# One-core attention and two feed-forward layers: six weight parts loaded and split between the loads of q and k, squares in PSUM, first chunks folded one by one

## What is computed

```python
qn = q / (norm(q, axis=1) + 1e-6); kn = k / (norm(k, axis=1) + 1e-6)   # over the tokens
s = kn.T @ qn / tau                       # 256 x 256
a = exp(s - s.max(-1)); a /= a.sum(-1) + 1e-9
x = v @ a                                 # 6016 x 256
h = x @ w_in
g = (a0 + a1*h + a2*h*h + a3*h**3) / (1 + |b0|*|h| + |b1|*h*h + 1e-6)
x = g @ w_out
h = x @ w2_in
out = (h * clip(h + 3, 0, 6) / 6) @ w2_out
```

## Time and profile before

| | |
|---|---|
| median of 3 runs | 1117.84 us (1117.04 to 1118.7) |
| profiled execution | 1118.82 us |
| its span, first to last instruction | 1117.0 us |
| mean granted TensorE clock | 0.995 |
| TensorE / VectorE / ScalarE / GpSimd busy | 98% / 80% / 78% / 70% |
| loads of q and k end, as TensorE sees it | 48.7 us |
| first `up1` ends, step 0 begins on ScalarE | 55.4 us |
| slot 16 begins on ScalarE | 108.7 us |

### The profile page before, as it was taken

How to read it: one execution, slowest core, us unless ns; L and a number is a source line. 1 busy time by engine, 2 the same in 40 slices (tenths; PEclk the granted TensorE clock), 3 DMA queues, 4 the chain that set the end, 5 groups by cost and what they waited for, 6 DMA issues and landing times.

```text
span 1117.0 us, 16082 instructions
## 1 busy us (share of the span) xinstructions
PE 1098.1 (98%) x5004; PEld 921.7 (83%) x5004; DVE 894.7 (80%) x1286; ACT 868.4 (78%) x1468; POOL 777.9 (70%) x625
## 2 busy tenths in 40 slices
PE   9988799999999999999999999999999999999998
PEld 8887688888888888888888888888888888888887
DVE  6689899987887887888888888888788798787632
ACT  6699888877877887887777877877877787777643
POOL 0279888777776677777777777777677777766643
PEclk9999899999999999999999999999999999999999
DMA  9931010010110010020011011011011010010010
GB/s 346 305 126 20 1 20 1 15 19 1 20 20 1 10 29 1 0 35 3 0 21 17 1 19 19 0 19 19 1 19 20 1 20 1 1 20 1 1 19 20
DMA packets 105465, 33.82 MB, mean 30 GB/s; under 512 B 92982, under 2 KB 98742, under 8 KB 105398
## 3 DMA queue, kind: packets, MB, share of 16 engines
q1 hardware_dynamic: 104832, 32.52, 11.6%
q10 hardware_dynamic: 566, 0.52, 0.1%
HBM read 26.87 MB, written 6.16 MB: 30 GB/s over the span
## 4 chain that ended last, share of the span: by engine, by line
PE 93%; DVE 3%; ACT 2%; POOL 1%; issue 1%; DMA 0%; SPq 0%; DVEq 0%; ACTq 0%
PE H L469 15%; PE H L471 15%; PE H L470 15%; PE YP L470 7%; PE YP L471 7%; PE YP L469 7%; PE OP L471 7%; PE OP L469 7%; PE OP L470 7%; PE OP L502 3%; PE OP L640 1%; PE OP L644 1%; PE OP L642 1%; DVE H L940 0%; ACT SQ L750 0%
## 5 line engine op out<-in xcount | busy, mean ns | idle before, releaser
L416 POOL TENSOR_TENSOR SQ<-SQ,AB 128x512 f32<-128x512 f32 x176 | 231.2, 1314 | 245.3 <-ACT SQ L750 245.0
L430 POOL TENSOR_TENSOR g_lo<-R,g_hi 128x512 fp32r<-128x512 f32 (+1 forms) x191 | 243.1, 1273 | 28.8 <-ACT g_hi L782 28.8
L422 POOL TENSOR_TENSOR g_lo<-SQ,Y 128x512 fp32r<-128x512 f32 (+1 forms) x192 | 244.9, 1276 | 6.1 <-DVE SQ L970 6.0
L748 ACT ACTIVATE AB<-H,absb 128x512 f32<-128x512 f32 x176 | 121.4, 690 | 142.7 <-PE H L471 142.7
L933 DVE TENSOR_TENSOR T<-T,H 128x512 f32<-128x512 f32 (+1 forms) x192 | 129.1, 672 | 79.2 <-ACT T L756 78.5
L948 DVE SCALAR_TENSOR_TENSOR g_hi<-H,coef,Y 128x512 fp32r<-128x512 f32 (+1 forms) x192 | 141.5, 737 | 58.1 <-ACT Y L769 57.3
L469 PE MATMUL H<-vT_hi,wf_hi 128*128 128x512 f32 (+1 forms) x384 | 149.9, 390 | 8.8 <-DVE SQ L970 4.7
L976 DVE SCALAR_TENSOR_TENSOR R<-R,H 128x512 f32<-128x512 f32 (+1 forms) x192 | 128.1, 667 | 35.3 <-ACT R L775 35.2
L775 ACT ACTIVATE R<-H 128x512 f32<-128x512 f32 (+1 forms) x192 | 113.4, 591 | 51.9 <-PE H L471 51.0
L469 PE MATMUL YP<-g_hi,wd_hi 128*128 128x512 f32 (+1 forms) x384 | 149.5, 389 | 3.6 <-POOL g_lo L422 2.6
L471 PE MATMUL H<-vT_hi,wf_lo 128*128 128x512 f32 (+1 forms) x384 | 148.8, 388 | 0.0
(11 more groups left out here) (107 smaller groups left out, 2085.4 us busy)
## 6 DMA issues: line engine op xcount, KB each, us to landing
qk<-in_q SPq DMA_DIRECT2D x22, 256.0 KB, 5.6
qk<-in_k SPq DMA_DIRECT2D x22, 256.0 KB, 6.2
v_blocks<-in_v SPq DMA_DIRECT2D x88, 64.0 KB, 2.2
out<-o_tok SPq DMA_DIRECT2D x80, 64.0 KB, 1.9
wd_raw<-in_moe_w_out SPq DMA_DIRECT2D x8, 512.0 KB, 9.1
w_raw_a<-in_moe_w_in SPq DMA_DIRECT2D x2, 1024.0 KB, 11.0
wu_raw<-in_moe_w_in SPq DMA_DIRECT2D x4, 512.0 KB, 6.2
qk<-in_q SPq DMA_DIRECT2D x3, 128.0 KB, 2.8
```

What stands on the lines that cost most here:

```text
L416: nc.gpsimd.tensor_tensor(SQ[:, j % 4, 0:w], SQ[:, j % 4, 0:w], AB[:, j % 2, 0:w], ALU.add)\
L422: nc.gpsimd.tensor_tensor(g1_lo[:, j % 4, 0:w], SQ[:, j % 4, 0:w], Y[:, j % 2, 0:w], ALU.mult)\
L430: nc.gpsimd.tensor_tensor(g2_lo[:, j % 4, 0:w], R[:, j % 2, 0:w], g2_hi[:, j % 4, 0:w].bitcast(fp32), ALU.subtract).then_inc(g2_lo_done, 1)
```

## The change

**Loads.** Six of the twelve parts come between the loads of q and k: wd1 part 0 behind load 4 and part 1 behind load 19, the four wu2 parts behind loads 7, 10, 13 and 16. ScalarE rounds each behind the next load's squares, and GpSimd makes the low halves as they come, no longer behind `square_rows_summed`. In step 0 wd1 parts 2 and 3 are split in slots 0 and 4, and no wu2 unit is left there; the eight wd2 units move from slots 11, 14, 16, 18, 19, 27, 29, 30 to 11, 12, 13, 16, 17, 18, 19, 29.

**Squares.** They go to two halves of PSUM `H`; the transposed block 0 of v therefore goes to `YP`, two loads later.

**Logits.** The product with both norms and the row maximum are one instruction; a 128x1 instruction negates the maximum.

**First chunks.** The first fold piece is made chunk by chunk: chunk 0 to `OP`, chunk 1 to `H`. VectorE makes both halves of chunk 0, ScalarE the high and VectorE the low half of chunk 1. The table load of `Abs_reciprocal_sqrt` comes ahead of that.

```diff
-    V0_LOADED, V0_TRANSPOSED, V0_SPLIT = 7, 10, 14
+    V0_LOADED, V0_TRANSPOSED, V0_SPLIT = 7, 12, 16
-    WU2_AT = 3, 5, 7, 8, 9, 12, 15, 17
-    WD2_AT = 11, 14, 16, 18, 19, 27, 29, 30
+    WD1_BEHIND, WU2_BEHIND = (4, 19), (7, 10, 13, 16)
+    WD1_AT = 0, 4
+    WD2_AT = 11, 12, 13, 16, 17, 18, 19, 29
...
-        squares = sb("squares", [P, 2, 2, QK, C], fp32, start)
...
+        def squares(n, m):
+            at = 2 * (n % 2)
+            return H[:, at:at + 2, 0:m * C].rearrange("p x (i c) -> p x i c", c=C)
...
+        def first_folded(i, c):
+            return (OP, H)[i][:, 2 * i + c, 0:P]
...
@@ sync: the loads
-            load_wd1(0)
-            load_wd1(1)
+                if n in WD1_BEHIND:
+                    load_wd1(WD1_BEHIND.index(n))
+                if n in WU2_BEHIND:
+                    load_wu2(WU2_BEHIND.index(n))
             load_w1(0)
             load_wd1(2)
+            load_wd1(3)
             load_w1(1)
-            load_wd1(3)
-            load_wu2(0)
             load_v(1)
-            for part in range(1, 4):
-                load_wu2(part)
...
@@ gpsimd
-            pool.wait_ge(square_rows_summed, 1)
-            for part in range(3):
-                wd1_split(part)
+            wd1_split(0)
+            for part in range(4):
+                wu2_split(part)
+            wd1_split(1)
...
@@ tensor
+            def fold_first():
+                pe.wait_ge(w1_in[0], 16)
+                for i in range(2):
+                    for c in range(CT):
+                        if i == 0:
+                            pe.wait_ge(probT_ready, c + 1)
+                        for d in range(CT):
+                            done = nc.tensor.matmul(first_folded(i, c), probT[:, d, c * P:(c + 1) * P],
+                                                    w_raw_a[:, d, i * P:(i + 1) * P], start=(d == 0),
+                                                    stop=(d == CT - 1))
+                        done.then_inc(first_made, 1)
...
-            fold(0)
+            fold_first()
...
@@ scalar
+                if n - 1 in WD1_BEHIND:
+                    wd1_round(WD1_BEHIND.index(n - 1))
+                if n - 1 in WU2_BEHIND:
+                    wu2_round(WU2_BEHIND.index(n - 1))
...
-            wd1_round(0)
-            wd1_round(1)
             act.wait_ge(norms_summed, 1)
             nc.scalar.activation(roots, sums, ACT.Sqrt).then_inc(roots_taken, 1)
-            wd1_round(2)
...
-            fold_split(0)
-            nc.scalar.activation(small[:, 40:41], root_b1, ACT.Abs_reciprocal_sqrt)
+            nc.scalar.activation(small[:, 40:41], ones[:, 0:1], ACT.Abs_reciprocal_sqrt)
+            act.wait_ge(sums_inverted, 1)
+            for c in range(CT):
+                act.wait_ge(first_made, CT + c + 1)
+                nc.scalar.activation(wf_hi[:, c, P:2 * P], first_folded(1, c), ACT.Identity,
+                                     scale=inverse_sum[:, c:c + 1]).then_inc(first_hi, 1)
...
@@ vector
-                link(nc.vector.scalar_tensor_tensor(prob[:, c, :], OP[:, c, 0:C], by_k[:, c:c + 1], spread,
-                                                    ALU.mult, ALU.mult))
-                nc.vector.tensor_reduce(small[:, 24 + c:25 + c], prob[:, c, :], AX.X, ALU.max, negate=True)\
+                link(nc.vector.tensor_tensor_reduce(prob[:, c, :], OP[:, c, 0:C], spread, by_k[:, c:c + 1], LOWEST,
+                                                    ALU.mult, ALU.max, small[:, 42 + c:43 + c]))
+                nc.vector.tensor_scalar(small[:, 24 + c:25 + c], small[:, 42 + c:43 + c], -1.0, None, ALU.mult)\
```

More of the change, by code:

```diff
@@ L274, in wait_h2, with wu2_part, wd1_rows @@
                 wait_chunk(engine, g2_done, back(blk, j, 2))
-        def wu2_unit(u):
-            at = u // 2 % 2 * F + u // 4 * (F // 2) + u % 2 * UNIT
-            return slice(at, at + UNIT)
+        def wu2_part(part):
+            half, c = part // 2, part % 2
+            return c, slice(half * F // 2, (half + 1) * F // 2)
+        def wd1_rows(part):
+            return slice(part * J // 4, (part + 1) * J // 4)
         def wd2_unit(u):
@@ L301, in load_wd1 @@
             def load_wd1(part):
-                rows = slice(part * J // 4, (part + 1) * J // 4)
+                rows = wd1_rows(part)
                 sp.dma_start(wd1_raw[:, rows, :], w_down_h[0][:, rows, :]).then_inc(wd1_in[part], 16)
@@ L309, in load_wu2 @@
             def load_wu2(part):
-                half, c = part // 2, part % 2
-                cols = slice(half * F // 2, (half + 1) * F // 2)
+                c, cols = wu2_part(part)
                 sp.dma_start(wu2_raw[:, c, cols], w_up_h[1][:, c, cols]).then_inc(wu2_in[part], 16)
@@ L386, in wd1_split, with wu2_split @@
             def wd1_split(part):
-                rows = slice(part * J // 4, (part + 1) * J // 4)
+                rows = wd1_rows(part)
                 pool.wait_ge(wd1_hi_done, part + 1)
                 low_half(wd1_lo[:, rows, :], wd1_raw[:, rows, :], wd1_hi[:, rows, :]).then_inc(wd1_lo_done, 1)
-            def wu2_split(u):
-                lo, raw, hi = (x[:].rearrange("p a b -> p (a b)")[:, wu2_unit(u)] for x in (wu2_lo, wu2_raw, wu2_hi))
-                pool.wait_ge(wu2_hi_done, u + 1)
-                low_half(lo, raw, hi).then_inc(wu2_lo_done, 1)
+            def wu2_split(part):
+                c, cols = wu2_part(part)
+                pool.wait_ge(wu2_hi_done, part + 1)
+                low_half(wu2_lo[:, c, cols], wu2_raw[:, c, cols], wu2_hi[:, c, cols]).then_inc(wu2_lo_done, 1)
             def wd2_split(u):
@@ L471, in split_product, with keep_clock @@
                 return nc.tensor.matmul(psum, w_lo, x_hi, start=False, stop=last)
-            def keep_clock(n):
+            def keep_clock(n, psum):
                 for _ in range(n):
-                    nc.tensor.matmul(H[:, 3, 0:P], ones[:], ones[:], start=True, stop=True)
+                    nc.tensor.matmul(psum, ones[:], ones[:], start=True, stop=True)
             def norms():
@@ L680, in wd1_round, with wu2_round @@
             def wd1_round(part):
-                rows = slice(part * J // 4, (part + 1) * J // 4)
+                rows = wd1_rows(part)
                 act.wait_ge(wd1_in[part], 16)
                 nc.scalar.activation(wd1_hi[:, rows, :], wd1_raw[:, rows, :], ACT.Copy).then_inc(wd1_hi_done, 1)
+            def wu2_round(part):
+                c, cols = wu2_part(part)
+                act.wait_ge(wu2_in[part], 16)
+                nc.scalar.activation(wu2_hi[:, c, cols], wu2_raw[:, c, cols], ACT.Copy).then_inc(wu2_hi_done, 1)
             for n, (_, m) in enumerate(loads):
@@ L818, in step @@
                         c2(*u2)
[L819 to L822 removed]
+                    if slot(t, j) in WD1_AT:
+                        wd1_round(2 + WD1_AT.index(slot(t, j)))
                     if slot(t, j) in WD2_AT:
@@ L871, in _ @@
                 nc.vector.tensor_tensor(square_sum[:, :, 0:m, :], square_sum[:, :, 0:m, :],
-                                        squares[:, n % 2, :, 0:m, :], ALU.add).then_inc(qk_summed, 1)
+                                        squares(n, m), ALU.add).then_inc(qk_summed, 1)
                 if n == COEF_USED + 1:
@@ L922, in fold_split @@
                         wf_hi[:, c, columns(n)].bitcast(fp32), ALU.mult, ALU.subtract).then_inc(fold_lo, 1)
-            fold_split(0)
+            dve.wait_ge(sums_inverted, 1)
+            for i in range(2):
+                for c in range(CT):
+                    cols = slice(i * P, (i + 1) * P)
+                    if i == 0:
+                        dve.wait_ge(first_made, c + 1)
+                        link(nc.vector.tensor_scalar(wf_hi[:, c, cols], first_folded(i, c), inverse_sum[:, c:c + 1], None,
+                                                     ALU.mult))
+                    else:
+                        dve.wait_ge(first_hi, c + 1)
+                    nc.vector.scalar_tensor_tensor(wf_lo[:, c, cols], first_folded(i, c), inverse_sum[:, c:c + 1],
+                                                   wf_hi[:, c, cols].bitcast(fp32), ALU.mult, ALU.subtract)\
+                      .then_inc(first_lo, 1)
             def horner_2(t, j):
```

61 lines of the change are left out of this document (26 added, 35 removed).

## The result

| | before | after |
|---|---|---|
| median of 6 runs each | 1118.05 us (1117.04 to 1118.7) | 1123.51 us (1122.55 to 1124.38) |
| after / before | | 1.005 (95% interval 1.0039 to 1.006) |
| profiled execution, its span | 1118.82, 1117.0 us | 1123.23, 1121.4 us |

The change made the kernel slower by 5.5 us, 0.5%. That is outside the predicted range (1114.5 to 1122).

The account below looks back on a forecast made before the run. TensorE is busy without a gap from 140 us, so only the loads, softmax and first fold, and slots 0 to 18 count: 4.4 - 0.7 - 1.6 - 0.9 = +1.2 us, median 1119.0 us, range 1114.5 to 1122.

Parts of the forecast that it names:

- transfers, at `norms()`: Loads: six early weight parts delay load 24 to 44.8 us and the row sum to 48.1 us; +4.4 us.
- rival 3: Loads: TensorE's clock falls after the new wait of about 2 us at `norms()`; +2.1 us, 1121.1 us in all, chance 0.22.
- softmax and first fold: Before slot 0: the maximum comes with the product, and two TensorE waits in the first fold go; -0.7 us.
- splits moved, slots 0 to 15: Step 0: slots shorten where units leave ScalarE, down to VectorE's pace; -1.6 us (0 to -4.0).
- splits moved, slots 16 to 21: Forecast for slots 16 to 18: GpSimd no longer late, TensorE's wait 3.6 instead of 4.51 us; -0.9 us.
- The price between the two rows: Loads: a wd1 part costs 1.6 us of transfer, between 1.29 us by bytes and 1.99 us by a measured stretch.
- it keeps up, but behind load 20 it starts late; I add 0.2 us: Loads, ScalarE: three loads and a rounding take 4.2 us against 5.2 us of transfers; only 0.2 us added.
- slots 8 and 9: Step 0: without their wu2 units this pair falls from 6.70 to VectorE's 6.04 us; 0.66 us gained.
- the end of the step: Slots 12 to 15: 12.0 us instead of 12.51, as 14 and 15 carry no unit; 0.5 us gained.
- slots 2 to 7: Step 0: units leave slots 3, 5 and 7, a wd1 part enters slot 4; some 0.4 us gained.
- rival 4: Step 0 gains nothing: ScalarE-VectorE waits set its pace, GpSimd stays late in slot 16; +3.7 us, 1121.5 us, chance 0.1.
- the product for slot 15 then waits only for VectorE's quotient: Slot 16: with no unit in slots 14 and 15 GpSimd is not late; its product ends 0.9 us earlier.

Follow-up runs that it names:

- e1: The changed kernel with its loads, roundings and splits of weights put back to the places of the kernel before; 1116.97 us, 0.9993.
- e9: The changed kernel with its six early transfers in place and its six roundings moved behind the exponentials; 1131.67 us, meant to be read at `norms()`.
- e5: The changed kernel with the rounding of wd1 part 1 moved from behind load 20's square to behind the last load's square; 1125.76 us, 1.0067.
- e3: The changed kernel with 12 more matmuls of a constant in TensorE's wait ahead of `norms()`; 1121.66 us, 1.0033.
- e2: The kernel before with only the six early loads, roundings and splits and the new slots; squares stay in SBUF; 1130.24 us, 1.0108.
- e4: The changed kernel with only wu2 parts 0 to 2 early; wd1 behind load 24, wd2 in the slots of before; 1119.91 us, 1.0014.

## Why the prediction failed

Set against e1, which shares all but the early parts, each term reads:

| term | predicted | measured |
|---|---|---|
| transfers, at `norms()` | +4.4, with 0.2 for roundings | +4.51 (e9 - e1) |
| roundings on top | in the above | +0.67 (after - e9) |
| clock behind the wait | 0 (rival 3: +2.1) | +1.76 (6.94 up to slot 0, less 5.18) |
| softmax and first fold | -0.7 | -0.88 (e1 - before) |
| splits moved, slots 0 to 15 | -1.6 | +0.04 |
| splits moved, slots 16 to 21 | -0.9 | -0.46 |
| sum | +1.2 | +5.6 |

**Right: the transfers.** The step from 19.65 us, 13 loads at 1.29 us, four parts at 1.29 and two at 1.6 gave 44.8 us for load 24; the square of that load begins at 44.97 in e9. The price between the two rows, 1.6 us for a wd1 part, held: behind load 4 the next load's square begins 3.12 us later in the changed kernel and 2.77 in e9, behind load 19 2.66 us later in e9, which leaves 1.4 to 1.8 us for the part. That TensorE's slack of 1.0 us goes, and that GpSimd's splits are hidden, held as well, the latter only because of the squares in PSUM. Right too: softmax and first fold. The fold rested on two waits that would go, and they went: from its start to slot 0 it takes 3.25 us in e1 instead of 3.86, the 0.6 I had forecast.

**Wrong, the step "it keeps up, but behind load 20 it starts late; I add 0.2 us".** The roundings cost 0.67 us beyond the transfers. The rounding at 40.96 us pushes the square of load 21, and from 42.95 us on VectorE's sums stand back to back. They are 1.3 us apart and the transfers 1.25 to 1.33, so what is late once stays late. But e5, which takes just that rounding away, ends the sums only 0.26 us sooner: there the squares wait for their transfers, and that of load 24 begins at 45.44, 0.47 us later than in e9. Why the transfers land later there stays open.

**Wrong, the clock (the chance, not the size).** I had it as a rival at 0.22 with 2.1 us; it cost 1.76 (e3 gives 1.66 of it back) and came in every profile in which TensorE waited 2.4 us or more at that place (after, e2, e5, e9). The one profile with a wait of 1.80 us (e4) has none, which makes no threshold, as seven other executions of e4 were at the lower clock for longer. Nor is 1.76 us the price each time: from `norms()` to slot 0, e2 and e5 lose 2.70 and 3.03 us. The forecast took a wait "some 2 us" long, by its own numbers 2.1 to 2.6, and set the clock's cost at nothing, as the fall that I had in mind stood behind a wait of 4.51 us. But the earlier trace rows show another fall in 60 to 70 us, behind waits of 1.19 us and less. A new wait with matmuls right behind it, all of them on the path, should have carried the fall in its price. With it the sum would have been near +3, slower by more than 0.2%.

**Wrong, the steps on the slots.** This is the largest error, 2.1 us, and the profile after hides it: slots 0 to 16 took 52.00 us instead of 53.22, near the 1.6 I had forecast. But e1, with no unit moved, takes 51.96. What before had lost there was the clock fall at 66 us, 1.29 us in slot 4, and it is gone in both. The units themselves give, after against e1: slots 8 and 9 gain 0.49 of the 0.66, the end of the step 0.2 of the 0.5, and slots 2 to 7, where I had 0.4 gained, lose 0.7, since slot 4 alone loses 0.94. In e1 ScalarE waits for nothing in slots 0 to 15. Where a unit goes, it now waits for VectorE's product (0.24 us in slot 7, 0.44 in slot 9) or GpSimd's low half (0.37 in slot 15), so a slot does not fall to VectorE's 2.63 us. In slot 4 I had only counted that a wd1 part comes in; the rounding of 1.07 us at 76.09 stands in ScalarE's queue, which is busy 3.97 of the 4 us from 76 to 80, so it lengthens the slot nearly by its own length. e4 has no part there, and its slot 4 takes 3.20 us as in e1 and slots 0 to 16 gain 0.85. I weighed the moved units by the engine they free, VectorE's 2.63 us a slot, and not this one by the engine it loads.

At slot 16 I had GpSimd no longer late, and the root 0.9 us sooner. ScalarE still waits 1.44 us for it (1.91 before). It is not the three splits in slots 11 to 13, as rival 4 has it: GpSimd idles just ahead. Its timeline in the profile after:

```profile
114.13 1.02 POOL L434 TENSOR_TENSOR g_lo<-SQ,Y 128x384 fp32r<-128x384 f32 x1 [0.73 <-DVE SQ L1008]
115.11 1.01 POOL L422 TENSOR_TENSOR SQ<-SQ,g_hi 128x384 f32<-128x384 f32 x1
116.08 1.26 POOL L428 TENSOR_TENSOR SQ<-SQ,AB 128x512 f32<-128x512 f32 x1
```

VectorE's quotient for slot 15 ends at 114.58, 1.1 us into slot 16, as I had it. But the low half of slot 14 stands ahead of the product in GpSimd's order and had to wait for VectorE's rest, so the product begins 1.61 us into the slot (2.06 before). The step that failed is "the product for slot 15 then waits only for VectorE's quotient". So 0.46 us came of the 0.9, and TensorE's wait there did not shrink.

Why the sum of terms, 5.6 us, is near the medians' 5.46: both are made against executions without the fall at 66 us. The profiled one of before has it, so that the two profiled spans lie only 4.4 us apart.
